# Reciprocals of the gate norms as one Newton step on a ScalarE guess

## What is computed

```python
mag = np.sqrt(a_re * a_re + a_im * a_im)
scale = np.minimum(mag, 0.999) / (mag + 1e-06)
a_re_n, a_im_n = (a_re * scale, a_im * scale)
for t in range(S):                      # S = 768, state D x D per head, D = 48
    new_re = ar * S_re - ai * S_im
    new_im = ar * S_im + ai * S_re
    S_re, S_im = (new_re + k[t] v[t]^T, new_im)
    y[t] = q[t] @ S_re
...
h = x @ w_in                            # 3072 tokens, 384 -> 2048 -> 384
g = np.maximum(h, 0.0) + alpha * np.minimum(h, 0.0)
x = g @ w_out
...                                     # then 8 experts, top-1, 384 -> 1024 -> 384
```

## Time and profile before

| | us |
|---|---|
| median of 3 runs | 968.17 (966.34 to 971.03) |
| the profiled execution | 968.83 |
| its span, first to last instruction | 966.9 |
| granted TensorE clock, mean | 0.922 of full |
| PE busy | 751.7 |
| DVE busy | 699.2 |
| ACT busy | 367.4 |

### The profile page before, as it was taken

The page is one execution under the profiler, slowest core; times in us unless marked ns, Lnnn a source line. Parts: engine busy times, 40 slices in busy tenths (PEclk is TensorE's granted clock), DMA queues, the critical chain, the costliest instruction groups (busy, mean ns, idle before and its releaser), DMA issues. The chain is left out here.

```text
span 966.9 us, 16131 instructions
## 1 busy us (share of the span) xinstructions
PE 751.7 (78%) x5478; PEld 723.3 (75%) x5479; DVE 699.2 (72%) x1231; ACT 367.4 (38%) x805; POOL 51.8 (5%) x48
## 2 busy tenths in 40 slices
PE   1343456987897989889798889979999547998786
PEld 1333456987886989788688788879999447998786
DVE  6967988988999799898899989875333373434333
ACT  5452234435434534433453353334433222322221
POOL 1000000000000000000000000000000012233122
PEclk9999567999999899999999999999999857999799
DMA  6542343243342424424242352233210393324520
GB/s 188 178 152 79 93 118 90 64 130 113 80 109 62 139 65 115 126 66 133 70 118 73 100 151 63 70 113 97 57 56 1 133 357 110 126 73 163 205 82 17
DMA packets 82433, 104.74 MB, mean 108 GB/s; under 512 B 15990, under 2 KB 68384, under 8 KB 82336
## 3 DMA queue, kind: packets, MB, share of 16 engines
q1 hardware_dynamic: 80544, 99.69, 35.2%
q0 software_dynamic: 1792, 3.76, 1.2%
HBM read 61.04 MB, written 12.19 MB: 76 GB/s over the span
## 5 line engine op out<-in xcount | busy, mean ns | idle before, releaser
L524 PE MATMUL out_ps<-w_out_hi,g_parts 128*128 128x394 f32 x768 | 225.3, 350 | 26.3 <-DVE g_parts L933 26.3
L514 PE MATMUL mlp_ps<-xT,w_in_hi 128*128 128x384 f32 x768 | 207.1, 351 | 20.3 <-DMA xT<-y_parts 8.6
L524 PEld LDWEIGHTS out_ps<-w_out_hi,g_parts 128*128 128x128 f32 x768 | 145.9, 193 | 30.3 <-DVE g_parts L933 30.2
L514 PEld LDWEIGHTS mlp_ps<-xT,w_in_hi 128*128 128x128 f32 x768 | 140.5, 194 | 27.5 <-issue 13.5
L928 DVE SCALAR_TENSOR_TENSOR g<-mlp_ps,slope_side,bent 128x384 f32<-128x384 f32 x128 | 78.6, 615 | 83.4 <-ACT bent L666 75.3
L524 PE MATMUL out_ps<-w_out_lo,g_parts 128*128 128x394 f32 x384 | 133.8, 348 | 0.0
L514 PE MATMUL mlp_ps<-xT,w_in_lo 128*128 128x384 f32 x384 | 131.2, 342 | 0.0
L666 ACT ACTIVATE bent<-mlp_ps,bend_size 128x384 f32<-128x384 f32 x128 | 73.7, 576 | 149.5 <-PE mlp_ps L514 149.0
L1303 PE MATMUL mlp_ps<-xT_e,w_sb 128*128 128x128 f32 x624 | 79.5, 290 | 19.3 <-issue 14.1
L1303 PEld LDWEIGHTS mlp_ps<-xT_e,w_sb 128*128 128x128 f32 x624 | 77.4, 205 | 22.1 <-issue 16.9
L672 ACT ACTIVATE g_parts<-g 128x384 fp32r<-128x384 f32 x128 | 66.2, 517 | 35.4 <-DVE g L928 35.4
(11 more groups left out here) (150 smaller groups left out, 1082.8 us busy)
## 6 DMA issues: line engine op xcount, KB each, us to landing
kq<-qk_dec SPq DMA_DIRECT2D x96, 144.0 KB, 3.0
w_sb<-in_w SPq DMA_DIRECT2D x8, 1536.0 KB, 7.7
w_raw<-in_w SPq DMA_DIRECT2D x8, 1536.0 KB, 12.0
gates<-in_a SPq DMA_DIRECT2D x24, 384.0 KB, 4.3
qk_raw<-in_qk SPq DMA_DIRECT2D x24, 384.0 KB, 4.2
xT<-y_parts SPq DMA_DIRECT2D x48, 144.0 KB, 2.8
v_nat<-in_v SPq DMA_DIRECT2D x24, 192.0 KB, 4.0
out<-x SPq DMA_DIRECT2D x8, 576.0 KB, 3.2
```

Of the source, the lines that this page charges most:

```text
L514: last = pe.matmul(ps[:, 0:HT], w_in_v[s][:, kk, f * P:(f + 1) * P], xT[n.p][:, kk, m, :], start=(kk == 0 and j == 0), stop=(kk == KT - 1 ...
L524: last = pe.matmul(out_ps[i][:, 0:DL], g_parts[:, f % 4, s, i * P:(i + 1) * P], w_out_v[m][:, f, :], start=(f == 0 and j == 0), stop=(f == ...
```

## The change

Both reciprocals of each chunk leave DVE. In their place ACT forms a guess of the reciprocal as exp(-ln x), and DVE refines it with one Newton step. `pad_gates` is gone; `log_gates` takes ln(norm + 1e-6) and `guess_gates` takes exp of its negative. `scale_gates` has three `scalar_tensor_tensor` in place of a reciprocal and one, and its product with the gates is a `scalar_tensor_tensor` too, which takes back the sign. For the second reciprocal ACT gains `log_inverse` and `guess_inverse`, and `inverse` is a product and a `scalar_tensor_tensor`. Each ln and exp is called for the three chunks in a row.

```diff
-                dve.wait_ge(norm_eps, val(g_ + 1))
-                dve.reciprocal(s1, s0).then_inc(norm_inv, 1)
-                dve.wait_ge(norm_inv, val(g_ + 1))
-                dve.scalar_tensor_tensor(out=s0, in0=size, scalar=0.999, in1=s1, op0=ALU.min,
+                dve.wait_ge(norm_guess, val(g_ + 1))
+                dve.scalar_tensor_tensor(out=s1, in0=size, scalar=1e-6, in1=s0, op0=ALU.add,
+                                         op1=ALU.mult).then_inc(norm_step, 1)
+                dve.scalar_tensor_tensor(out=s0, in0=size, scalar=0.999, in1=s0, op0=ALU.min,
+                                         op1=ALU.mult).then_inc(norm_step, 1)
+                dve.wait_ge(norm_step, val(g_ * 2 + 2))
+                dve.scalar_tensor_tensor(out=s1, in0=s1, scalar=2.0, in1=s0, op0=ALU.subtract,
                                          op1=ALU.mult).then_inc(norm_scale, 1)
...
             def inverse(h, c):
-                dve.wait_ge(f_summed, val(g_ + 1))
-                dve.reciprocal(of_chunk(inv[:, :], c), of_chunk(norms[:, :], c)).then_inc(f_inverted, 1)
+                s0, s1 = of_chunk(sq[:, 0, :], c), of_chunk(sq[:, 1, :], c)
+                dve.wait_ge(f_guess, val(g_ + 1))
+                dve.tensor_tensor(s1, of_chunk(norms[:, :], c), s0, ALU.mult).then_inc(f_step, 1)
+                dve.wait_ge(f_step, val(g_ + 1))
+                dve.scalar_tensor_tensor(out=of_chunk(inv[:, :], c), in0=s1, scalar=2.0, in1=s0, op0=ALU.subtract,
+                                         op1=ALU.mult).then_inc(f_inverted, 1)
...
+            def log_inverse(h, c):
...
+                act.wait_ge(f_summed, val(g_ + 1))
+                act.activation(of_chunk(sq[:, 0, :], c), of_chunk(norms[:, :], c), ACT.Ln,
+                               scale=2.0 ** 63).then_inc(f_log, 1)
+
+            def guess_inverse(h, c):
...
+                act.wait_ge(f_log, val(g_ + 1))
+                act.activation(s0, s0, ACT.Exp, bias=shift[:, 0:1], scale=-1.0).then_inc(f_guess, 1)
```

The order of the calls is changed too. On ACT, in `step`:

```diff
-                    pad_gates(nxt, 0)
                 of_mlp(2)
                 high_y(h, 0)
                 if more:
-                    pad_gates(nxt, 1)
+                    log_gates(nxt, 0)
+                    log_gates(nxt, 1)
+                    log_gates(nxt, 2)
                 of_mlp(3)
-                if more:
-                    pad_gates(nxt, 2)
                 scale_state(h, 0)
-                of_mlp(4, 5)
+                if more:
+                    guess_gates(nxt, 0)
+                    guess_gates(nxt, 1)
+                of_mlp(4)
+                if more:
+                    guess_gates(nxt, 2)
+                of_mlp(5)
```

More of the change, by code:

```diff
@@ L732, in step @@
                     square_products(nxt, 1)
+                    square_products(nxt, 2)
                     take_factors(nxt)
-                    square_products(nxt, 2)
-                of_mlp(15, 16)
+                of_mlp(14)
+                if more:
+                    for c in range(NC):
+                        log_inverse(nxt, c)
+                of_mlp(15)
+                if more:
+                    for c in range(NC):
+                        guess_inverse(nxt, c)
+                of_mlp(16)
                 if mlp_too:
@@ L756, in _ @@
                 root_gates(Half(0, 0), c)
-            act.wait_ge(bias_made, 1)
+            act.wait_ge(bias_made, 2)
             act.wait_ge(alpha_made, 5)
             for c in range(NC):
-                pad_gates(Half(0, 0), c)
+                log_gates(Half(0, 0), c)
+            for c in range(NC):
+                guess_gates(Half(0, 0), c)
             for kind, n in WEIGHT_ORDER:
@@ L768, in _ @@
             take_factors(Half(0, 0))
+            for c in range(NC):
+                log_inverse(Half(0, 0), c)
+            for c in range(NC):
+                guess_inverse(Half(0, 0), c)
             act.wait_ge(wo_lo, NF)
@@ L803, in scale_gates @@
                 at = of_chunk(gates[h.p][:, :, :], c)
-                dve.tensor_tensor(at, at, s0.unsqueeze(1).broadcast_to([P, 2, DM]), ALU.mult).then_inc(a_normed, 1)
+                dve.scalar_tensor_tensor(out=at, in0=at, scalar=-1.0, in1=s1.unsqueeze(1).broadcast_to([P, 2, DM]),
+                                         op0=ALU.mult, op1=ALU.mult).then_inc(a_normed, 1)
             def multiply(h, done, x, y_re, y_im, new_re, new_im, prod_a, prod_b):
@@ L878, in decay_qk @@
                 k_ = qk_raw[:, m, :, 1, :]
-                dve.tensor_tensor(k_, k_, tiles(of_chunk(inv[:, :], c)), ALU.mult).then_inc(k_scaled, 1)
+                dve.scalar_tensor_tensor(out=k_, in0=k_, scalar=-1.0, in1=tiles(of_chunk(inv[:, :], c)), op0=ALU.mult,
+                                         op1=ALU.mult).then_inc(k_scaled, 1)
                 if back(h, c):
@@ L958, in step @@
                 of_mlp(2)
-                if more:
-                    scale_gates(nxt, 0)
                 low_y(h, 0)
@@ L963, in step @@
                 of_mlp(3)
-                if more:
-                    scale_gates(nxt, 1)
                 of_mlp(4)
@@ L968, in step @@
                 if more:
-                    scale_gates(nxt, 2)
+                    scale_gates(nxt, 0)
+                    scale_gates(nxt, 1)
                 of_mlp(5)
@@ L972, in step @@
                 if more:
[L973 removed]
+                    scale_gates(nxt, 2)
                 of_mlp(6)
                 if more:
+                    within(nxt, 1)
                     within(nxt, 2)
[L977 removed]
                 of_mlp(7)
@@ L1001, in step @@
                 of_mlp(12)
+                low_y(h, 2)
+                add_state(h, 2)
                 if more:
                     carry_products(nxt, 0)
-                low_y(h, 2)
-                add_state(h, 2)
                 of_mlp(13)
```

47 lines of the change are left out of this document (29 added, 18 removed).

## The result

The changed kernel takes 1014.86 us (median, 1013.08 to 1018.22), the kernel before 968.16 us (966.34 to 971.03). The ratio is 1.049, with a 95% interval of 1.046 to 1.052: slower by 4.9%. The profiled execution has a span of 1012.1 us against 966.9.

The account below looks back on a forecast made before the run. Bound: DVE's way from the first mask to the next half's decay_qk, then the moves. 968.8 + 46 (preamble 3, step 0 5.3, six steps 38) + 6 for the clock = 1021, forecast 1020 us, range 988 to 1047.

Parts of the forecast that it names:

- The bound: Each step: DVE from the first mask to decay_qk of the next half, then the moves, 7.6 us to PE.
- DVE's terms: On DVE, Newton steps for reciprocals: 8.6 us less a half, some 69 us over eight halves.
- ACT's terms: On ACT, Ln and Exp at 524 and 603 ns, a table load 1.28 us, four blocks of 2.8 us a step.
- The far end of 0.8 us: On ACT, slowest value allowed for each ln and exp instead of 0.5: 3 us a step more, 1040 us.
- The waits: DVE waits for ACT in slots 3, 4, 14 and 15 and at low_g(15): 1.9, 4.3, 3.1, 1.25, 2.65 us.
- the clock's term: At six step boundaries, TensorE between its two levels after a 5 us wait: 0 to 12 us, taken as 6.
- The preamble: Before the steps, loads, ln and exp delay the inverse's end from 71.9 to 74.9: +3.0 us.
- The six steps: Steps 1 to 6, each 6.3 us longer from gains 5.8, costs 1.0 and 11 of waiting: 38 us.
- (a): Faster, about 935 us: waits don't grow and 4.8 us a step is gained at seven boundaries; chance 0.11.
- (b): Table loads between activations hidden, three of 1.28 us leave each step's way: about 992 us; chance 0.12.
- (c): Loads amid PSUM reads wait for the queue to empty and cost double: about 1048 us; chance 0.07.
- (d): No change: PE's pace mostly swallows the waits in slots 3 and 4, tail costs only inverses' savings; chance 0.05.

Follow-up runs that it names:

- The front taken alone: Changed kernel with ln, exp, Newton and order kept for the scales, but inverse and the step's last part as before the change: 969.41 us, ratio 1.002.
- the tail taken alone: Kernel before with only the changed inverse and last part (squares ahead of slot 14, ln, exp, Newton, decay_qk behind slot 16): 1016.9 us, ratio 1.051.
- the kernel without guesses: Kernel before, own order, with Newton steps on DVE replacing both reciprocals and no ln or exp on ACT, so reciprocals are not computed: 907.3 us, ratio 0.938.

## Why the prediction was right

**The bound.** The claim was that a step is DVE's way from the first mask to `decay_qk`, and then the moves. It held: over step 1 the way grew by 5.95 us and the boundary behind it by 1.89, 7.84 in all, and the step grew by 7.84. The front taken alone left the way within 0.2 us a step and the time within 0.6%, the tail taken alone made it 5.8 us a step longer and the time 5.1%. One limit shows in the kernel before: at the end of step 2 PE began the turns without a wait for kq (at 320.24, 11.27 us behind `decay_qk`), so there PE was the last and not kq. In the changed kernel PE waits for kq at all six boundaries.

**DVE's terms.** One half less by 8.6 us was 69 us in all, and 68.2 came. The products that turned from tensor_tensor into scalar_tensor_tensor were bounded to nothing, and are: 958 ns at L852, as much as the tensor_tensor of the kernel before (958 at L804).

**ACT's terms.** Ln and Exp were taken at 524 and 603 ns from the earlier trace rows. The groups of ACT by line in the changed kernel (busy, mean ns | idle before):

```profile
L620 ACT ACTIVATE sq<-norms,tiny 128x384 f32<-128x384 f32 x24 | 13.0, 606 | 0.1
L642 ACT ACTIVATE sq<-sq,shift 128x384 f32<-128x384 f32 x24 | 13.0, 605 | 0.1
...
L634 ACT ACTIVATE sq<-norms 128x384 f32<-128x384 f32 x24 | 11.5, 521 | 2.7 <-DVE norms L912 2.6
L628 ACT ACTIVATE sq<-sq 128x384 f32<-128x384 f32 x24 | 11.4, 514 | 0.1
...
L628 ACT ACT_TABLE_LOAD x8 | 10.3, 1283 | 0.1
```

The far end of 0.8 us was not needed. A load is 1.28 us everywhere, 41 of them.

**The waits.** Forecast 1.9, 4.3, 3.1, 1.25 and 2.65, measured 1.88, 4.18, 2.97, 1.06 and 2.68. The wait for kq at the start of step 2 was forecast at 5.0 and is 4.19; kq came when it was forecast, and PE was ready 0.7 us later. From the carry products on, `decay_qk` takes 15.05 us (224.90 to 239.95), where 15.1 were forecast. This is what walking two in-order queues against each other gives, with durations that the trace has.

**The sizes that were off.** Up to the mark of step 7 the sum was 46 us without the clock's term, 52 with it, and 47.1 came. The preamble was put at 3.0 and is 1.2 (88.49 against 87.29 at the mark of step 0); step 0 was put at 5.3 and is 5.2. The six steps were put at 38 and 6 for the clock, 44, and are 40.7. Taken apart by the two timelines, over six steps:

| | forecast | before | after | difference |
|---|---|---|---|---|
| mask to the end of `decay_qk` (DVE's way) | 38 | 421.8 | 453.5 | +31.7 |
| end of `decay_qk` to the turns | 0 | 51.7 | 48.5 | -3.1 |
| start of the turns to the second mask | 6 | 17.0 | 29.2 | +12.2 |

So the clock's term was half of what came, and the way's was 6 us too large: I walked step 1, whose way grew by 5.95, and the others' grew by 3.9 to 7.3, which makes 5.3 in the mean of all six. The turns take 1.75 us at the last five boundaries, as at the lower level in the earlier trace rows, and from their start to the second mask it is 4.75 to 5.23 us there against 2.8 to 2.9. That the sum of these three came out within 4 us is in part luck, since their errors have opposite signs; the mechanism, waits on the way and a slower TensorE behind the wait, is what the rows show. Behind the last mark it is 1.9 us less than before, which the sum didn't have; the load for the exponential in `phase2` is gone, which by its length would be 1.28 of it. The wait for kq over the whole kernel, "some 85 us or more", is 103.8. The six boundaries have it as counted, 32.0 us against 3.4 before; what I left out is that PE waits longer in the preamble and step 0 too, 13.5 us more over their four waits.

**The rivals.** (a), faster by 34 us, had about the right price for what DVE saves: the kernel without guesses has 37.8 us at the last mark. What it lacked was its condition. New waits ahead of `decay_qk` had to stay under 4.8 us a step. The five in step 1 come to 12.8, and less those that are gone it is some 11, as counted. (b), loads off the way, 28 us less: without loads it is 28.8 less at the last mark, so this is what they cost, and they are on the way. (c), loads that cost double, falls with the gaps of 0.01 and 0.02 us on the two sides of a load, right behind a PSUM read too (167.75 to 167.76, 169.04 to 169.06), and with the 3.83 us a step that taking three loads off the way gave. The drain that the Trainium skill, "ScalarE: Activation LUTs", section "What ACT_TABLE_LOAD costs", states is not in these rows, and the time of 1057 us that it gave is 42 too high. (d), a tail that costs only what the inverses save, falls with the tail taken alone.

## What to carry to other kernels

Before work goes to an engine that is idle half of the time, read what stands behind the new place in its in-order queue, and who waits for that: here the four blocks of ln and exp cost 6.7 us of waiting a step on the engine that they were to relieve by 5.8. Part of a wait is the order alone: of the 4.18 us of slot 4 the kernel in the same order but without the blocks keeps 2.09. A saving counts only where it lies ahead of what ends last, and the cheapest guess was the one that replaced work of ACT (the root and the pad) instead of adding to it. An experiment that changes values must be read at a mark ahead of everything that depends on values.
